# The second chunk's bonus on the diagonal of its scores, and its inverse scan fed from PSUM in two halves

## The chip, the core and the metric

The kernel runs on one core of a Trainium2 chip. The metric is the device time of one execution in microseconds (us), taken as the median of several executions. The core has a matrix engine (TensorE, PE in the rows; its weight loads are PEld), a vector engine (VectorE, DVE), a scalar engine (ScalarE, ACT), GpSimd (POOL), and SyncE (SP), whose queue issues the loads. They share an SBUF memory; TensorE writes to PSUM, which is in 8 banks and which VectorE and ScalarE can read and write too.

## The reference

Three layers in a row: a linear attention with decays and a bonus `u`, a dense ELU layer, and a layer of 4 experts.

```python
def _attn_ref(r, k, v, w, u):          # B, H, S, D = 2, 8, 768, 48
    for t in range(S):
        kt, vt, rt, wt = (k[:, :, t], v[:, :, t], r[:, :, t], w[:, :, t])
        cur = np.einsum('bhd,bhe->bhde', u[None] * kt, vt)
        y[:, :, t] = np.einsum('bhd,bhde->bhe', rt, state + cur)
        state = wt[:, :, :, None] * state + np.einsum('bhd,bhe->bhde', kt, vt)
...
def _moe_ref(x, w_in, w_out):          # 1536 tokens, 384 -> 2048 -> 384
    h = x @ w_in
    g = np.where(h > 0.0, h, alpha * (np.exp(np.minimum(h, 0.0)) - 1.0))
    return (g @ w_out).astype(np.float32)
...
def _moe2_ref(x, domain_probs, w1, w2):  # 4 experts, 384 -> 1024 -> 384
    p = domain_probs / (domain_probs.sum(-1, keepdims=True) + 1e-09)
    for e in range(E):
        h = np.maximum(x @ w1[e], 0.0)
        out += p[:, e:e + 1] * (h @ w2[e])
```

## The kernel before

The 1536 tokens are 12 chunks of 128. For a chunk, VectorE scans the decays forward (`products`, L840), takes the reciprocal of the last product of each of 8 segments (L843, `inv_end`), and scans backward from them (`inverses`, L849). The results scale k and r (`scale_k` L858, `scale_r` L865). TensorE makes the scores of 8 heads (`scores`, L1141) into two banks, one for even and one for odd heads; VectorE masks them into `att` (L878); TensorE multiplies `att` with v, first the even heads (L1220), then the odd ones (L1224, L1228), which gives the attention's output y, transposed. ScalarE rounds it into `x_hi` (L680, L689) and VectorE takes the remainder into `x_lo` (L907, L917). The matrix products of the layers are each three passes over such high and low parts (L1288 to L1290).

The bonus adds, to each token's y, its v times a number for each head: the sum over d of r, k and u. For chunks 2 to 11 that number is written on the diagonal of `att`: GpSimd multiplies r, k and u (L494, L498), VectorE sums them (L897), GpSimd writes the diagonal (`bonus_diagonal`, L506), and VectorE lays the masked scores beside it (L881). The first two chunks go another way: GpSimd multiplies r and k (L583), TensorE multiplies that with `u_blk`, in which `u` fills 48 columns for each head (`bonus`, L1182, 4 matmuls of 96 columns, each in two passes), VectorE multiplies v with the result (`bonus_v`, L903), and TensorE transposes this product into y (`turn_bonus`, L1195). `u_blk` is made by ScalarE (L704) from the 4 columns of `u_col`.

Chunks 0 and 1 stand ahead of everything; they are the tokens of the first, 256 wide tile of the ELU layer. This layer is a loop of steps n, 16 for each of 4 tiles. Step n makes 128 of the 2048 hidden values with `up(n)` (9 matmuls), ScalarE takes relu and exp (L737, L739), VectorE ends the ELU (`elu`, L953), ScalarE rounds (`hi_g`, L745), VectorE takes the remainder (`lo_g`, L959), and TensorE runs `down1(n)` two steps later, so its order is up(2), down1(0), up(3), down1(1) and so on. Between them come the later chunks, by tables of steps (`SCORES`, `PRODUCTS`, `SCALE_K` and so on): chunk 2's scores are in step 8, chunk 3's in step 12.

During the first tile the weights are rounded as well. Slice n (a tuple `(n, half)`: half 0 is for `up(n)`, half 1 for `down1(n)`) lands in `raw`; ScalarE makes `w_hi` (whole slices L693, halves L698 in the order of `HI_BETWEEN`), and the remainder `w_lo` is made by GpSimd (L517, two pieces of 192 columns for each half, in the order of `LO_POOL`) or by VectorE (L924, `LO_VECTOR`). `up(n)` waits for its slice's `w_lo`. GpSimd's order is fixed: the two r times k products, 11 halves (22 pieces), the bonus terms of chunk 2, the half (9, 0), the diagonal of chunk 2, five halves, the bonus terms of chunk 3, and so on. It begins the 22 pieces when chunk 1's r is scaled:

```python
            pool.wait_ge(s_qp, FIRST)
```

At the start TensorE also runs matmuls on zeros (`warm`, L1257; `fill`, L1262), which keep it busy and clear banks. After the four tiles come the experts, which TensorE runs through with the other engines feeding it.

## Time and profile before

| what | value |
|---|---|
| median of 3 executions | 652.43 us (652.41 to 652.44) |
| the profiled execution's own time | 652.4 us |
| its span in the trace | 650.6 us |
| granted TensorE clock, mean | 1.00 of full speed |
| TensorE matmul busy | 644.9 us (99%) |
| VectorE / ScalarE / GpSimd busy | 415.0 / 242.9 / 295.5 us |

The span is the time from the first to the last instruction in the trace; the execution's own time has 1.8 us around it. Busy time of TensorE counts matmuls from issue to modelled end, and they overlap, so a start time tells more than a share.

### The profile page before, as it was taken

To read this page: it belongs to the slowest core of one execution; us is meant where nothing else is said; L and a number is where in the kernel's file an instruction comes from. 1 tells how busy PE (TensorE), PEld (TensorE's weight loads), DVE (VectorE), ACT (ScalarE), POOL (GpSimd) and SP (SyncE) were. 2 spreads that over 40 slices of the span, in tenths; PEclk is the share of its full clock that TensorE was granted. 3 is DMA by queue.
4 is the path that set the end of the run, shared out by engine and by line. 5 is a ranking of instruction groups with operands and counts; after the bars stand their busy time and mean duration, and the time that the engine had idled before them with its cause. 6 is when DMAs were issued, how large, how long until landed. Compare 5 with 4: busy or idle time off the path is not lost.

```text
span 650.6 us, 13114 instructions
## 1 busy us (share of the span) xinstructions
PE 644.9 (99%) x4727; PEld 597.6 (92%) x4727; DVE 415.0 (64%) x775; ACT 242.9 (37%) x569; POOL 295.5 (45%) x370
## 2 busy tenths in 40 slices
PE   8999999999999999999999999999999999999998
PEld 5999999787888888999999999999999999999997
DVE  7888887865347666656565656565656565656564
ACT  4786656655435555322222222222222222222221
POOL 4897422520299999998009900009910019000000
PEclk9999999999999999999999999999999999999999
DMA  8933234200000133100012100013100011001011
GB/s 326 404 124 111 87 101 158 85 3 2 2 1 1 50 98 97 50 2 1 0 49 98 49 2 0 0 49 98 49 0 0 0 49 49 1 1 48 0 50 48
DMA packets 13280, 38.09 MB, mean 59 GB/s; under 512 B 1968, under 2 KB 4016, under 8 KB 13232
## 3 DMA queue, kind: packets, MB, share of 16 engines
q1 hardware_dynamic: 12944, 37.03, 16.2%
q8 instruction: 33, 0.54, 0.3%
q10 hardware_dynamic: 288, 0.39, 0.2%
q14 instruction: 15, 0.12, 0.1%
HBM read 35.06 MB, written 2.36 MB: 58 GB/s over the span
## 4 chain that ended last, share of the span: by engine, by line
PE 96%; DVE 2%; issue 1%; ACT 1%; DMA 0%; DVEq 0%; ACTq 0%
PE bank L1288 30%; PE bank L1289 30%; PE bank L1290 30%; PE bank L1141 2%; PE bank L1208 1%; PE bank L1220 1%; PE bank L1164 1%; PE bank L1152 1%; DVE fr L840 1%; DVE fr L849 0%; DMA rkw<-rkw_dram 0%; PE bank L1224 0%; PE bank L1228 0%; DVE bank L953 0%; PE bank L1195 0%
## 5 line engine op out<-in xcount | busy, mean ns | idle before, releaser
L1288 PE MATMUL bank<-x_lo,w_hi 128*128 128x256 f32 (+2 forms) x416 | 137.8, 331 | 0.0
L1289 PE MATMUL bank<-x_hi,w_lo 128*128 128x256 f32 (+2 forms) x416 | 135.2, 325 | 0.0
L1290 PE MATMUL bank<-x_hi,w_hi 128*128 128x256 f32 (+2 forms) x416 | 135.2, 325 | 0.0
L1289 PE MATMUL bank<-w_hi,g_lo 128*128 128x384 f32 x384 | 129.6, 337 | 0.0
L1290 PE MATMUL bank<-w_hi,g_hi 128*128 128x384 f32 x384 | 129.3, 337 | 0.0
L1288 PE MATMUL bank<-w_lo,g_hi 128*128 128x384 f32 x384 | 129.0, 336 | 0.0
L803 ACT ACTIVATE g_hi<-bank 128x512 fp32r<-128x512 f32 x96 | 57.5, 599 | 144.3 <-DVE bank L1009 122.4
L1288 PEld LDWEIGHTS bank<-x_lo,w_hi 128*128 128x128 f32 x416 | 78.3, 188 | 8.0 <-issue 0.4
L1290 PEld LDWEIGHTS bank<-x_hi,w_hi 128*128 128x128 f32 x416 | 78.2, 188 | 7.4
L1289 PEld LDWEIGHTS bank<-x_hi,w_lo 128*128 128x128 f32 x416 | 78.3, 188 | 7.1
L1002 DVE TENSOR_TENSOR u_sum<-p_copy,bank 128x256 f32<-128x256 f32 x56 | 23.6, 421 | 92.5 <-ACT p_copy L725 91.8
L529 POOL TENSOR_TENSOR raw<-raw 128x128 f32<-128x128 f32 x16 | 7.4, 463 | 157.7 <-DMA raw<-w_dram 157.7
L1288 PEld LDWEIGHTS bank<-w_lo,g_hi 128*128 128x128 f32 x384 | 72.2, 188 | 0.0
L1290 PEld LDWEIGHTS bank<-w_hi,g_hi 128*128 128x128 f32 x384 | 72.1, 188 | 0.0
L1289 PEld LDWEIGHTS bank<-w_hi,g_lo 128*128 128x128 f32 x384 | 72.0, 188 | 0.0
L725 ACT COPY p_copy<-bank 128x256 f32<-128x256 f32 x56 | 21.0, 375 | 134.4 <-PE bank L1290 134.3
L1082 DVE SCALAR_TENSOR_TENSOR g_lo<-bank,g_hi 128x512 fp32r<-128x512 f32 x96 | 65.9, 686 | 7.1 <-ACT g_hi L803 6.8
L1288 PE MATMUL bank<-g_lo,w_hi 128*128 128x256 f32 (+1 forms) x192 | 65.3, 340 | 0.2 <-DVE g_lo L959 0.2
L1290 PE MATMUL bank<-g_hi,w_hi 128*128 128x256 f32 (+1 forms) x192 | 64.9, 338 | 0.0
L1289 PE MATMUL bank<-g_hi,w_lo 128*128 128x256 f32 (+1 forms) x192 | 64.7, 337 | 0.0
L953 DVE SCALAR_TENSOR_TENSOR bank<-neg,bank 128x256 f32<-128x256 f32 (+1 forms) x64 | 35.9, 561 | 42.2 <-ACT neg L739 42.0
L541 POOL TENSOR_TENSOR w_lo<-raw,w_hi 128x768 fp32r<-128x768 f32 x32 | 58.6, 1853 | 0.0
(132 smaller groups left out, 1274.1 us busy)
## 6 DMA issues: line engine op xcount, KB each, us to landing
raw<-w_dram SPq DMA_DIRECT2D x48, 384.0 KB, 3.7
rkw<-rkw_dram SPq DMA_DIRECT2D x10, 772.5 KB, 5.2
tok<-tok_dram SPq DMA_DIRECT2D x10, 576.0 KB, 6.6
out_dram<-acc SPq DMA_DIRECT2D x10, 192.0 KB, 1.9
rkw<-rkw_dram SPq DMA_DIRECT2D x2, 512.0 KB, 4.1
rkw<-rkw_dram SPq DMA_DIRECT2D x2, 260.5 KB, 3.1
tok<-tok_dram SPq DMA_DIRECT2D x2, 192.0 KB, 4.9
out_dram<-acc ACTq DMA_DIRECT2D x2, 192.0 KB, 1.9
```

The costliest lines, as they stand in the source:

```text
L529: pool.tensor_tensor(s1, a21, a22, ALU.add).then_inc(s_ws, 1)
L541: pool.tensor_tensor(w_lo[:, slot, :], raw[:, slot, :], w_hi[:, slot, :].bitcast(F32), ALU.subtract).then_inc(s_w, 1)
L725: act.copy(p_copy[:, 0, :], bank[6][:, 0:QUARTER]).then_inc(s_pc, 1)
L803: act.activation(g2[0][:, p % 2 * 2 + o, :], bank[o][:, :], ACT.Relu).then_inc(s_gh, 1)
L840: dve.tensor_tensor_scan(fr[:, 0:SCAN], rkw[c % DEEP][:, 2 * NRK:2 * NRK + SCAN], reset[:, :], 0.0, ALU.mult, ALU.add).then_inc(s_f, 1)
L953: dve.scalar_tensor_tensor(out=h, in0=neg[:, k, 0:w], scalar=-1.0, in1=h, op0=ALU.add, op1=ALU.max).then_inc(s_elu, 1)
L1002: dve.tensor_tensor(u2, p1, p6, ALU.add).then_inc(s_u2, 1)
L1082: dve.scalar_tensor_tensor(out=g2[1][:, r, :], in0=bank[o][:, :], scalar=0.0, in1=g2[0][:, r, :].bitcast(F32), op0=ALU.max, op1=ALU.subtra ...
L1141: ins = pe.matmul(banks["x"][o][:, cols], k[rows, cols], q[rows, cols], start=True, stop=True)
L1288: pe.matmul(out, wh, ml, start=start, stop=False, skip_group_check=shared)
L1289: pe.matmul(out, wl, mh, start=False, stop=False, skip_group_check=shared)
L1290: return pe.matmul(out, wh, mh, start=False, stop=stop, skip_group_check=shared)
```

## The change

For chunk 1 the bonus goes on the diagonal of `att` too. TensorE's `bonus` now multiplies with `u_col` itself, which has 2 columns for each pair of heads (the 96 column blocks and `u_blk` are gone), so it yields 8 numbers for each token. ScalarE copies chunk 1's 8 numbers to `bonus_sb` and writes the four even heads' diagonals (`even_diagonals`); GpSimd writes the odd heads' ones in one instruction, ahead of its 22 pieces. VectorE then lays the masked scores beside them with four predicated copies of 256 columns in place of two multiplications of 512, the first two pairs of heads ahead of the last two; the scores of the last two pairs go to banks 6 and 7. `turn_bonus` and `bonus_v` remain for chunk 0 alone, and `values_by_block` follows the masks' order. Chunk 0's y keeps its way.

Chunk 1's reciprocals go to banks 0 and 1, and its inverse scan reads them there, in two scans of 260 columns. GpSimd's second r times k product now waits for the first of these only. Chunk 2's inverse scan, which was one scan at the end of step 3, becomes two, at the end of steps 3 and 4.

Slice 5's `w_hi` is no longer made whole ahead of the steps, but in halves in steps 0 and 1, and what followed moves by a half up to step 2. The order of GpSimd's first halves becomes (0, 0), (1, 0), (0, 1), (1, 1). The fills at the start are one more, and go to other banks.

```diff
-INVERSES = {FIRST: 3}
+FIRST_INVERSES = {FIRST: 3}
...
-LO_POOL = [(n, half) for n in range(J1) for half in range(2) if (n, half) not in LO_VECTOR + LO_LAST] + LO_LAST
+LO_AHEAD = [(0, 0), (1, 0)]
+LO_POOL = LO_AHEAD + [(n, half) for n in range(J1) for half in range(2)
+                      if (n, half) not in LO_AHEAD + LO_VECTOR + LO_LAST] + LO_LAST
...
-HI_FIRST = 6
-HI_BETWEEN = {1: ((6, 0), (6, 1)), 2: ((7, 0),), 3: ((7, 1), (8, 0)), 4: ((8, 1),), 5: ((10, 0),),
+HI_FIRST = 5
+HI_BETWEEN = {0: ((5, 0),), 1: ((5, 1), (6, 0)), 2: ((6, 1), (7, 0)), 3: ((7, 1), (8, 0)), 4: ((8, 1),), 5: ((10, 0),),
...
-            u_col = sb("u_col", [P, PAIRS], scope=scope)
-            u_blk = sb("u_blk", [P, PAIRS, PD], scope=scope)
+            u_col = sb("u_col", [P, PAIRS, 2], scope=scope)
...
-            bonus_v_sb = sb("bonus_v_sb", [P, 2, DM], scope=scope)
+            bonus_v_sb = sb("bonus_v_sb", [P, DM], scope=scope)
...
+        BANKS0 = dict(x=bank[6:8], y=bank[2], yt=blocks_in(bank[2]), kt=bank[5], u=heads_in(bank[6], 0),
+                      bonus=bank[3][:, P:P + H])
+        BANKS1 = dict(x=bank[0:2], x_late=bank[6:8], yt=[bank[b][:, 0:P] for b in (4, 3, 5)], kt=bank[7],
+                      u=heads_in(bank[7], 0), bonus=bank[5][:, P:P + H])
+
+        ENDS1 = bank[0:2]
...
         def inverted(c):
 
-            return c + 1 + max(c - FIRST, 0)
+            return 2 * c + 1
+
+        def ended(c):
+
+            return c + 1 + min(c, 1)
...
-            sp.dma_start(const[:, :], const_d).then_inc(s_const, 16)
+            sp.dma_start(const[:, :], const_d[:, 0:C_BLK]).then_inc(s_const, 16)
...
+            def on_diagonal(c, o):
+
+                heads = bonus_sb[:, c % 2, :].rearrange("p (a o) -> p o a", o=2)
+                return pool.affine_select(att[:, o, :, :], heads[:, o, :].unsqueeze(2).broadcast_to([P, PAIRS, CH]),
+                                          pattern=[[0, PAIRS], [1, CH]], compare_op=ALU.is_equal, fill=0.0, base=0,
+                                          channel_multiplier=-1)
...
+            pool.wait_ge(s_first_bon, 1)
+            pool.wait_ge(s_val, 1)
+            on_diagonal(1, 1).then_inc(s_diag_odd, 1)
             pool.wait_ge(s_qp, FIRST)
             def lo_ws(halves):
...
+
+            def even_diagonals(banks):
+                act.wait_ge(s_pb, 2)
+                act.copy(bonus_sb[:, 1, :], banks["bonus"]).then_inc(s_first_bon, 1)
+                act.wait_ge(s_val, 1)
+                act.wait_ge(s_const, 16)
+                act.wait_ge(s_first_bon, 1)
+                for p in range(PAIRS):
+                    act.activation(att[:, 0, p, :], ident, ACT.Copy,
+                                   scale=bonus_sb[:, 1, 2 * p:2 * p + 1]).then_inc(s_diag_even, 1)
+
             copy_tail(0)
-            act.wait_ge(s_uc, 32)
-            act.wait_ge(s_const, 16)
-            for p in range(PAIRS):
-                act.activation(u_blk[:, p, :], blocks, ACT.Copy, scale=u_col[:, p:p + 1]).then_inc(s_ub, 1)
             copy_kt(0, BANKS0)
...
             hi_w(1)
             copy_odd(1)
             hi_w(2)
+            even_diagonals(BANKS1)
             hi_w(3)
             hi_x(0, BANKS0["y"])
-            hi_w(4)
             for k in range(KT):
                 hi_x_block(1, BANKS1["yt"], k)
-            hi_w(5)
+            hi_w(4)
...
-                dve.reciprocal(inv_end[:, SEG - 1:SCAN:SEG], fr[:, SEG - 1:SCAN:SEG]).then_inc(s_end, 1)
+                if c == 1:
+                    dve.wait_ge(s_clear, 2)
+                    for ends, first in zip(ENDS1, (0, SCAN // 2)):
+                        dve.reciprocal(ends[:, SEG - 1:SCAN // 2:SEG],
+                                       fr[:, first + SEG - 1:first + SCAN // 2:SEG]).then_inc(s_end, 1)
+                else:
+                    dve.reciprocal(inv_end[:, SEG - 1:SCAN:SEG], fr[:, SEG - 1:SCAN:SEG]).then_inc(s_end, 1)
 
             def inverses(c, part=0, parts=1):
 
-                dve.wait_ge(s_end, c + 1)
+                dve.wait_ge(s_end, ended(c))
                 n = SCAN // parts
+                if c == 1:
+                    ends = backwards(ENDS1[1 - part], n - 1, TILE, n)
+                else:
+                    ends = backwards(inv_end, SCAN - 1 - part * n, SCAN, n)
                 dve.tensor_tensor_scan(backwards(fr, 2 * SCAN - 1 - part * n, 2 * SCAN, n),
                                        backwards(rkw[c % DEEP], 2 * NRK + SCAN - part * n, RKW, n),
-                                       backwards(inv_end, SCAN - 1 - part * n, SCAN, n), 0.0,
+                                       ends, 0.0,
                                        ALU.mult, ALU.add).then_inc(s_fr, 1)
...
+
+            def mask_half(o, late, banks):
+
+                if late:
+                    dve.wait_ge(s_px, 2)
+                else:
+                    dve.wait_ge(s_px_first, 1)
+                if o == 0:
+                    dve.wait_ge(s_diag_even, 2 * late + 2)
+                else:
+                    dve.wait_ge(s_diag_odd, 1)
+                pairs = slice(2 * late, 2 * late + 2)
+                masks = mask.unsqueeze(1).broadcast_to([P, 2, CH])
+                found = banks["x_late" if late else "x"][o][:, :].rearrange("p (a t) -> p a t", a=PAIRS)[:, pairs, :]
+                dve.copy_predicated(att[:, o, pairs, :], masks.bitcast(I32), found).then_inc(
+                    s_att if late else s_att_first, 1)
...
+            def bonus_v(banks):
+                dve.wait_ge(s_pb, 1)
+                landed(dve, s_tok, 0)
+                heads = v_of(0).rearrange("p (h d) -> p h d", h=H)
+                dve.tensor_tensor(bonus_v_sb[:, :].rearrange("p (h d) -> p h d", h=H), heads,
+                                  banks["bonus"].unsqueeze(2).broadcast_to([P, H, D]), ALU.mult).then_inc(s_cv, 1)
...
             products(1)
-            inverses(1)
+            inverses(1, 0, 2)
+            inverses(1, 1, 2)
             dve.wait_ge(s_const, 16)
             mask_scores(0, 0, BANKS0)
             mask_scores(0, 1, BANKS0)
             scale_k(1)
             scale_r(1)
-            bonus_v(0, BANKS0)
-            bonus_v(1, BANKS1)
-            mask_scores(1, 0, BANKS1)
-            mask_scores(1, 1, BANKS1)
+            bonus_v(BANKS0)
+            for late in range(2):
+                for o in range(2):
+                    mask_half(o, late, BANKS1)
...
-                for c in due(n, 0, INVERSES):
-                    inverses(c)
+                for part in range(2):
+                    for c in due(n, part, FIRST_INVERSES):
+                        inverses(c, part, 2)
...
                         rows, cols = slice(64 * o, 64 * o + D), slice(p * CH, (p + 1) * CH)
-                        ins = pe.matmul(banks["x"][o][:, cols], k[rows, cols], q[rows, cols],
-                                        start=True, stop=True)
+                        x = banks["x_late"] if c == 1 and p >= 2 else banks["x"]
+                        ins = pe.matmul(x[o][:, cols], k[rows, cols], q[rows, cols], start=True, stop=True)
+                    if c == 1 and p == 1:
+                        ins.then_inc(s_px_first, 1)
                 ins.then_inc(s_px, 1)
...
-                pe.wait_ge(s_ub, PAIRS)
-                if c == 1:
-                    pe.wait_ge(s_kt, 1)
+                pe.wait_ge(s_uc, 32)
                 for p in range(PAIRS):
-                    ins = pe.matmul(banks["bonus"][:, p * PD:(p + 1) * PD], rk[:, c, p * CH:(p + 1) * CH], u_blk[:, p, :],
-                                    start=True, stop=True)
+                    ins = pe.matmul(banks["bonus"][:, 2 * p:2 * p + 2], rk[:, c, p * CH:(p + 1) * CH], u_col[:, p, :],
+                                    start=False, stop=True, skip_group_check=True)
                 ins.then_inc(s_pb, 1)
...
+            def turn_bonus(yt):
+
+                pe.wait_ge(s_cv, 1)
                 for k in range(KT):
-                    ins = pe.matmul(yt[k], bonus_v_sb[:, c % 2, k * P:(k + 1) * P], ident,
-                                    start=first and (k == 0 or c == 1), stop=True, is_transpose=first,
+                    ins = pe.matmul(yt[k], bonus_v_sb[:, k * P:(k + 1) * P], ident, start=False, stop=True,
                                     skip_group_check=True)
-                if not first:
-                    ins.then_inc(s_py, 1)
+                ins.then_inc(s_py, 1)
...
+            def values_by_block(yt):
+
+                landed(pe, s_tok, 1)
+                pe.wait_ge(s_att_first, 1)
+                for b in (0, 1, 3, 4):
+                    even_strip(1, yt, b)
+                pe.wait_ge(s_att_first, 2)
+                pe.wait_ge(s_odd, 2)
+                odd_strip(1, yt, 2)
+                odd_end(1, yt, 1).then_inc(s_y_first, 1)
+                odd_strip(1, yt, 5)
+                odd_end(1, yt, 4)
+                pe.wait_ge(s_att, 3)
+                for b in (6, 9, 7, 10):
+                    even_strip(1, yt, b)
+                pe.wait_ge(s_att, 4)
+                odd_end(1, yt, 7).then_inc(s_y_first, 1)
+                odd_strip(1, yt, 8)
+                odd_strip(1, yt, 11)
+                odd_end(1, yt, 10).then_inc(s_py, 1)
...
             pe.wait_ge(s_zero, 2)
-            warm(WARM_UP, 1)
+            warm(WARM_UP // 2, 0)
+            warm(WARM_UP - WARM_UP // 2, 1)
             pe.wait_ge(s_zero, 4)
-            fill(2, 1)
+            fill(1, 3)
+            fill(1, 4)
             scores(0, BANKS0)
             pe.wait_ge(s_const, 16)
             turn_k(0, BANKS0)
             bonus(0, BANKS0)
-            fill(1, 1)
-            fill(1, 2)
+            fill(2, 2)
+            pe.wait_ge(s_kt, 1)
+            fill(1, 5)
             values_even(0, BANKS0["yt"])
             values_odd(0, BANKS0["yt"], s_val)
             bonus(1, BANKS1)
             scores(1, BANKS1)
-            turn_bonus(0, BANKS0["yt"], False)
-            turn_bonus(1, BANKS1["yt"])
-            values_even(1, BANKS1["yt"])
-            values_odd_by_block(1, BANKS1["yt"])
+            turn_bonus(BANKS0["yt"])
+            values_by_block(BANKS1["yt"])
             update(0, BANKS0)
```

ScalarE before the loop and in its step 0, before:

```order
L652 COPY tail<-fr 128x4
L704 ACTIVATE u_blk<-const,u_col 128x96 x4
L647 COPY kt_sb<-bank 128x512
L652 COPY tail<-fr 128x4
L676 COPY v_odd<-tok 128x4x16
L693 CAST w_hi<-raw 128x768 x2
L676 COPY v_odd<-tok 128x4x16
L693 CAST w_hi<-raw 128x768 x2
L680 CAST x_hi<-bank 128x3x128
L693 CAST w_hi<-raw 128x768
L689 CAST x_hi<-bank 128x128 x3
L693 CAST w_hi<-raw 128x768
```

And now, from the second copy of `v_odd` up to step 0's rounding of g:

```order
L696 COPY v_odd<-tok 128x4x16
L713 CAST w_hi<-raw 128x768
L723 COPY bonus_sb<-bank 128x8
L728 ACTIVATE att<-const,bonus_sb 128x128 x4
L713 CAST w_hi<-raw 128x768
L700 CAST x_hi<-bank 128x3x128
L709 CAST x_hi<-bank 128x128 x3
L713 CAST w_hi<-raw 128x768
L764 ACTIVATE neg<-bank 128x256
L766 ACTIVATE neg<-neg 128x256
L667 COPY kt_sb<-bank 128x512
L718 CAST w_hi<-raw 128x384
```

The four activations of 96 columns at the start are gone; a copy of 8 columns and four activations of 128 columns stand between slice 2 and slice 3; of slices 4 and 5, one whole cast is left behind the `x_hi` casts, and a half of slice 5 stands in step 0.

GpSimd from its first product to the diagonal of chunk 2, before:

```order
L583 TENSOR_TENSOR rk<-rkw 128x512 x2
L517 TENSOR_TENSOR w_lo<-raw,w_hi 128x192 x22
L494 TENSOR_TENSOR tok<-tok 128x192 x2
L498 TENSOR_TENSOR tok<-tok,u_rep 128x192 x2
L517 TENSOR_TENSOR w_lo<-raw,w_hi 128x192 x2
L506 AFFINE_SELECT att<-bonus_sb 128x512 x2
```

And now:

```order
L600 TENSOR_TENSOR rk<-rkw 128x512 x2
L517 AFFINE_SELECT att<-bonus_sb 128x512
L534 TENSOR_TENSOR w_lo<-raw,w_hi 128x192 x22
L507 TENSOR_TENSOR tok<-tok 128x192 x2
L511 TENSOR_TENSOR tok<-tok,u_rep 128x192 x2
L534 TENSOR_TENSOR w_lo<-raw,w_hi 128x192 x2
```

One diagonal of 512 columns stands ahead of the 22 pieces; all else keeps its place behind it.

## Rows read from the trace of the kernel before

**Rows 1.** The page's first part: busy time, share and instructions of each engine.

```profile
PE 644.9 (99%) x4727; PEld 597.6 (92%) x4727; DVE 415.0 (64%) x775; ACT 242.9 (37%) x569; POOL 295.5 (45%) x370
```

**Rows 2.** Windows, 60 to 640 us: busy time by engine, clock, DMA share, GB/s.

```profile
60.00:640.00 580.00, 580.00 (x4059) 539.32 (x4058) 360.19 (x674) 201.25 (x457) 248.11 (x302) 1.00 0.12 39
```

**Rows 3.** The chain that ended last, up to 18 us: start, us, what.

```profile
11.11 0.67 DVE att L878
...
11.92 0.65 PE bank L1220 x16
...
13.07 1.06 PE bank L1182 x8
14.13 1.09 PE bank L1141 x16
15.22 1.19 PE bank L1195 x9
...
17.43 0.60 PE bank L1164 x16
```

**Rows 4.** VectorE's timeline at the head: start, us, instruction, operands.

```profile
5.19 1.24 DVE L849 TENSOR_TENSOR_SCAN fr<-rkw,inv_end 128x520 f32<-128x520 f32 x1
...
9.31 1.88 DVE L849 TENSOR_TENSOR_SCAN fr<-rkw,inv_end 128x520 f32<-128x520 f32 x1
...
13.12 0.68 DVE L865 TENSOR_TENSOR neg<-rkw,fr 128x512 f32<-128x512 f32 x1
```

**Rows 5.** GpSimd's timeline at the head.

```profile
7.91 2.19 POOL L583 TENSOR_TENSOR rk<-rkw 128x512 f32<-128x512 f32 x1 [5.04 <-DVE neg L865]
...
13.88 18.33 POOL L517 TENSOR_TENSOR w_lo<-raw,w_hi 128x192 fp32r<-128x192 f32 x22 [1.23 <-DVE neg L865]
```

**Rows 6.** TensorE's timeline: the two fills behind the first bonus matmuls.

```profile
11.06 0.71 PE L1262 MATMUL bank<-g_hi 128*128 128x512 f32 x2
```

**Rows 7.** Groups up to 60 us, by form: count, busy us, mean ns, idle before.

```profile
L881 DVE COPY_PREDICATED att<-const,bank 128x512 f32<-128x512 int32 x4 | 2.7, 730 | 0.0
...
L667 ACT ACTIVATE st<-st,alpha 128x96 f32<-128x96 f32 x8 | 2.3, 368 | 0.0
...
L652 ACT COPY tail<-fr 128x4 f32<-128x4 f32 x4 | 0.8, 198 | 3.0 <-DVE fr L840 2.8
...
L506 POOL TENSOR_SCALAR_AFFINE_SELECT att<-bonus_sb 128x512 f32<-128x512 f32 x4 | 2.4, 633 | 0.7 <-DVE bonus_sb L897 0.7
```

**Rows 8.** ScalarE's timeline around the first `up`.

```profile
16.12 0.48 ACT L680 CAST x_hi<-bank 128x384 fp32r<-128x384 f32 x1 [1.50 <-PE bank L1195]
16.50 0.84 ACT L693 CAST w_hi<-raw 128x768 fp32r<-128x768 f32 x1
...
20.67 0.37 ACT L745 CAST g_hi<-bank 128x256 fp32r<-128x256 f32 x1
```

**Rows 9.** Groups up to 60 us, by form: the casts of half a slice.

```profile
L698 ACT CAST w_hi<-raw 128x384 fp32r<-128x384 f32 x20 | 9.4, 504 | 0.0
```

**Rows 10.** Timelines of VectorE, then TensorE, around chunk 2's inverse scan.

```profile
28.45 1.69 DVE L849 TENSOR_TENSOR_SCAN fr<-rkw,inv_end 128x520 f32<-128x520 f32 x1
...
31.04 0.42 DVE L959 TENSOR_TENSOR g_lo<-bank,g_hi 128x256 fp32r<-128x256 f32 x1
...
31.08 0.28 PE L1290 MATMUL bank<-x_hi,w_hi 128*128 128x256 f32 x1
31.52 0.39 PE L1288 MATMUL bank<-g_lo,w_hi 128*128 128x256 f32 x1 [0.16 <-DVE g_lo L959]
```

**Rows 11.** Groups up to 60 us, by form: the inverse scans of 260 columns.

```profile
L849 DVE TENSOR_TENSOR_SCAN fr<-rkw,inv_end 128x260 f32<-128x260 f32 x4 | 2.8, 692 | 0.0
```

**Rows 12.** Timelines of GpSimd, then TensorE: half (9, 0) and `up(9)`.

```profile
36.00 1.59 POOL L517 TENSOR_TENSOR w_lo<-raw,w_hi 128x192 fp32r<-128x192 f32 x2
...
38.53 0.36 PE L1288 MATMUL bank<-x_lo,w_hi 128*128 128x256 f32 x1
```

**Rows 13.** Timelines of VectorE, then TensorE: half (14, 0) and `up(14)`.

```profile
50.58 0.55 DVE L897 TENSOR_REDUCE bonus_sb<-tok 128x8 f32<-128x384 f32 x1 [1.04 <-POOL tok L498]
51.05 0.42 DVE L953 SCALAR_TENSOR_TENSOR bank<-neg,bank 128x256 f32<-128x256 f32 x1
...
52.24 0.59 DVE L924 TENSOR_TENSOR w_lo<-raw,w_hi 128x384 fp32r<-128x384 f32 x1
...
53.41 0.29 PE L1288 MATMUL bank<-x_lo,w_hi 128*128 128x256 f32 x1
```

61 lines of the change are left out of this document (20 added, 41 removed).

## The prediction, made before the changed kernel ran

> **What bounds the kernel now.** First the page's first part: TensorE is busy for 644.9 of the span's 650.6 us [rows 1], and a window from 60 to 640 us has it busy in all 580 us, at a granted clock of 1.00, the 2.4 GHz level [rows 2]. There the reader sees that nothing behind 60 us can be won or lost but by matmuls, and the change removes none there. So the change is worth exactly the time by which TensorE's stream of `up` and `down1` reaches its steady part earlier or later. Then the chain that ended last, for the head: it goes through VectorE's first mask at 11.11, and from 11.92 to the end of chunk 0's update at 18.03 it lies on TensorE [rows 3]. `up(0)` starts at 17.99. Third, the timelines of the four engines up to 60 us, to find every wait of TensorE in the loop. There are two short ones: 0.2 us before `down1(0)`, which waits for step 0's `lo_g`, and one at 31.08, where a matmul is followed by the next at 31.52 although they elsewhere follow in 0.12; it waited for the `lo_g` at 31.04, and this for the scan of 1.69 us at 28.45 [rows 10]. Last, the slices: by how much each `w_lo` is done before the `up` that waits for it. That is the view on which my number hangs.
>
> The profiled execution took 652.4 us, 1.8 more than its span; the median is 652.43. I count shifts of TensorE's stream and add them to 652.4.
>
> **The inverse scan of chunk 1.** A scan of 520 columns takes 1.24 us when GpSimd is idle (at 5.19) and 1.88 at 9.31 [rows 4], while GpSimd's first product runs from 7.91 to 10.10 [rows 5]. The excess is 0.64, and 9.31 + 0.64 is about where GpSimd ends. The Trainium skill (SBUF — State Buffer, section "SBUF: two separate sides") says that a VectorE instruction with two SBUF inputs and a GpSimd instruction that reads SBUF take turns on a port pair for a whole instruction each; by it, a scan fed from PSUM has one SBUF input and waits for nothing, and the trace's 0.64 agrees. No row shows a scan fed from PSUM. Bounds: with the excess gone, two halves of 0.69 as later ones [rows 11], less 0.08 of overlap, behind two reciprocals that cost 0.1 more than one: VectorE gets to the first mask at about 10.75 in place of 11.11. With the excess staying it is 11.3. I take the first, but it makes no difference worth a name, because of what TensorE does. It ran two fills from 11.06, the second at 11.38 [rows 6], and now runs three of about 0.21 (the distance at the full clock, from these rows between 0.2 and 0.3), so that it is not free before 11.8, and the switch to the narrow matmuls of `values_even` adds 0.1: 11.9, as before. The mask is ready by then in both cases. Only the odd half comes sooner, since it no longer waits for the second mask: 0.1. VectorE's earlier `scale_r` (it ended at 13.80 [rows 4], now about 13.2) releases chunk 1's scores, which however stand behind the bonus matmuls on TensorE.
>
> **The bonus matmuls.** Eight passes took 1.06 us with 96 columns [rows 3], 0.13 each; `turn_bonus` did nine passes of 128 columns in 1.19, 0.13 each as well. A quarter fewer columns saved nothing, so the weights, 128 columns in both, set the pace. With 2 columns I take no saving; the other bound is that nearly all of 1.0 us goes. The Trainium skill (TensorE: Matmul & The Clock Gate, section "LDWEIGHTS (loading the stationary operand)") gives the load of 128 columns as 107 ns whatever follows, which would leave at most 0.02 us a pass to win. So chunk 1's bonus ends at 14.03 (14.13 - 0.1) and its scores run from 13.95 to 15.1.
>
> **The diagonals and masks.** ScalarE copies the 8 numbers (0.2, as the small copy of 198 ns) to 14.2, then writes four diagonals. The nearest rows are activations of 96 columns, 368 ns each [rows 7], which follow each other in 0.27; 128 columns give 0.29 and 0.39. The second ends at 14.9, the fourth at 15.5. GpSimd's diagonal takes 0.63 [rows 7] from 14.3. VectorE's predicated copies of 512 columns take 0.73 [rows 7]; of 256 columns, 0.46, one each 0.36. They start at 14.9, 15.3, 15.5 and 15.9 and end at 16.35. Before, the masks ended at 16.56. TensorE drops three of nine passes of `turn_bonus`, 0.35 us, and reaches the last odd heads at 16.4, chunk 0's update at 16.8 and `up(0)` at 17.4 (the update took 0.60 [rows 3]). But `up(0)` also waits for x. ScalarE's cast of slice 3, 0.84 a piece [rows 8], now stands behind the diagonals, 15.4 to 16.2; the `x_hi` casts, which started at 16.12 [rows 8], start at about 16.15, and slice 4's cast between them is gone, so that the `x_lo` of the first block is there at 17.4 in place of 17.84. I take `up(0)` at 17.55: 0.44 earlier. Bounds: 0.1 (if the diagonals cost 0.1 more each) and 0.8.
>
> **Steps 0 to 4.** ScalarE now casts half of slice 5 in step 0, 0.50 us by the group [rows 9], 0.40 of it in the queue, between `copy_kt` and `hi_g(0)`, which stood at 20.67 [rows 8]. With 0.44 - 0.40 it stands at about 20.5 to 20.65, and `elu(1)` is 0 to 0.15 earlier. `lo_g(0)` waited for VectorE's `add_update` and is 0.4 earlier, which TensorE's `down1(0)` gets. From there TensorE has no wait up to 31.08, so its lead is 0.35. Then chunk 2's scan: one half of 0.69 [rows 11] leaves step 3, so `lo_g(4)` is there by 0.6 to 1.0 earlier than 31.04 and TensorE's stall of 0.32 (31.52 less 31.08 less 0.12), with 0.1 of slower restart, is gone [rows 10]. The second half stands behind `lo_g(4)`; `lo_g(5)` was done 0.7 us before `down1(5)`, which covers it; uncovered it would cost 0.6. TensorE's lead at step 8 is then 0.35 + 0.42, about 0.75 us.
>
> **GpSimd, and where the lead goes.** Its 22 pieces started at 13.88 [rows 5]. Now a diagonal stands ahead of them, which waits for TensorE's bonus and ScalarE's copy: start 14.3, 0.6 in the queue, pieces from 14.9. That is 1.0 late, and GpSimd has no idle time between 13.88 and 50.5 in which to catch up. The order in front gives (1, 0) earlier, so the first steps are safe: (3, 0) was 2.5 us ahead of its `up`, (7, 0) 2.1. But (9, 0) ends at 36.00 + 1.59 = 37.59 and `up(9)` starts at 38.53 [rows 12]: 0.94 of slack, against a lateness of 1.0 plus TensorE's lead of 0.75. TensorE will wait there, and what remains of the lead is 0.9 less the lateness. The second place is behind it: VectorE sits idle for 1.04 us until GpSimd has chunk 3's bonus terms, at 50.58, and from there `elu`, `hi_g`, `lo_g` and half (14, 0) follow one another, to 52.24 + 0.59 = 52.83; `up(14)` starts at 53.41 [rows 13]. Slack 0.58, less 0.05 to hand over: 0.53. A lateness L gives TensorE's stream a shift of L - 0.53, later, unless that is under minus 0.75. L starts at 1.0. It changes by chance: 22 pieces of 0.59 alone took 18.33, the rest being turns with VectorE's scans and remainders, and two half scans in place of a whole one save GpSimd perhaps 0.2. Bounds for L at 50 us: 0.3 and 1.2. I take 0.65, so the shift is +0.1 and the time 652.5.
>
> **Rivals.**
> - The lead is carried (chance 0.27). GpSimd's lateness shrinks to 0.3 or less, because the bonus matmuls with 2 columns do come cheaper and its diagonal starts at 13.9, or because its turns with VectorE fall well. For it: what these turns cost it is a matter of phase (18.33 us against 22 x 0.67 [rows 5]). Time 652.4 - 0.2 to 0.8, 651.6 to 652.2.
> - Slower through GpSimd (0.16). L is 1.0 or more at 50 us. The mechanism is the one place `up(14)`, the price is L - 0.53, and it decides from L = 0.53 on; beyond 0.2% it needs L above 1.8, for which the diagonal would have to start at 15.1. Time 652.9 to 653.3.
> - The change does not do what it says (0.07): diagonals dearer than 0.5 us each put the masks at 17, `up(0)` is not earlier, only the stall at 31 goes, and GpSimd is late in addition. Time 652.3 to 653.
> - The forecast (0.50): `up(9)` and `up(14)` take the lead back; 652.2 to 652.8.
>
> **How the numbers follow.** A measurement of this kernel tells 0.2% from no change, 1.3 us, so the bounds are 651.1 and 653.7. The largest gain that the head and the stall hold is 0.8 + 0.42 = 1.2 us, still inside; the loss needs L above 1.8. So: same 0.93, faster 0.03, slower 0.04. The range for 8 in 10 takes the forecast and most of both neighbours: 651.6 to 653.0. Its lower end is the whole lead carried, 652.4 - 0.75, its upper end L of 1.1.
>
> **What the profile would show.** `values_even` of chunk 0 at 11.9 still, behind a third fill; eight bonus passes still near 1.0 us; an inverse scan of 260 columns at 9.4 with no excess; masks ending near 16.35; `up(0)` near 17.55; `hi_g(0)` near 20.6; no gap at 31. GpSimd's 22 pieces from 14.9; a wait of TensorE before `up(9)`, for GpSimd, and one before `up(14)`, for VectorE. If TensorE waits at neither, I am wrong in L and the time is below 652. If `up(0)` is at 18 or later, I am wrong in the diagonals.

## The result, and the profile after

The changed kernel takes 653.41 us, the median of 20 executions (653.12 to 655.03), against 652.45 us for the kernel before, measured beside it (20 executions, 652.35 to 652.54). The ratio is 1.0017, with a 95% interval of 1.001 to 1.0023. That is 0.96 us more, still inside the 0.2% named in the prediction, but outside its range, and the forecast was 652.5.

The first profiled execution took 654.88 us and had a low TensorE clock for 3.4 us at the head (it is shown further down, for its clock). The rows of this section are from another execution of the same kernel, with the clock at 1.00: 653.35 us, span 651.5, where before had 652.4 and 650.6.

First the page's first part and the window from 60 to 640 us. They answer to [rows 1] and [rows 2].

```profile
PE 645.1 (99%) x4725; PEld 597.8 (92%) x4725; DVE 414.7 (64%) x779; ACT 243.3 (37%) x571; POOL 295.9 (45%) x371
...
60.00:640.00 580.00, 579.95 (x4058) 539.03 (x4058) 360.54 (x675) 201.48 (x457) 248.99 (x303) 1.00 0.12 39
```

TensorE reads as full behind 60 us, as before, but for 0.05 us. Waits of 0.1 or 0.2 us hide under the modelled ends in this view, so the starts are read from here on. TensorE's timeline at the head:

```profile
10.20 1.05 PE L1238 MATMUL bank<-u_col,rk 128*128 128x2 f32 x8 [0.59 <-POOL rk L600]
11.12 0.96 PE L1328 MATMUL bank<-g_hi 128*128 128x512 f32 x3
12.00 0.64 PE L1268 MATMUL bank<-att,tok 128*32 128x128 f32 x16
...
14.00 1.16 PE L1198 MATMUL bank<-neg,tok 48*128 48x128 f32 x16
...
17.24 0.67 PE L1222 MATMUL bank<-tok,kt_sb 128*64 128x48 f32 x16
17.84 0.39 PE L1355 MATMUL bank<-x_lo,w_hi 128*128 128x256 f32 x1
```

From the start of chunk 1's eight bonus passes to the start of its scores it is 0.98 us now (13.02 to 14.00), where it was 1.06 with 96 columns [rows 3]: 0.08 less for eight passes. (The 1.05 in the row counts the last pass to its modelled end.) Chunk 0's values start at 12.00 behind three fills. Chunk 0's update starts 0.12 earlier than before, at 17.24 for 17.36 on the same timeline, and `up(0)` starts at 17.84, only 0.15 before the 17.99 of before. VectorE, then ScalarE, then GpSimd at the head:

```profile
9.41 1.28 DVE L886 TENSOR_TENSOR_SCAN fr<-rkw,bank 128x260 f32<-128x260 f32 x2
10.61 1.26 DVE L912 TENSOR_TENSOR att<-bank,const 128x512 f32<-128x512 f32 x2
...
15.18 1.45 DVE L931 COPY_PREDICATED att<-const,bank 128x256 f32<-128x256 int32 x4 [1.65 <-ACT att L728]
```
```profile
14.11 0.17 ACT L723 COPY bonus_sb<-bank 128x8 f32<-128x8 f32 x1 [0.73 <-PE bank L1238]
14.39 1.28 ACT L728 ACTIVATE att<-const,bonus_sb 128x128 f32<-128x128 f32 x4
```
```profile
7.96 3.60 POOL L600 TENSOR_TENSOR rk<-rkw 128x512 f32<-128x512 f32 x2 [5.08 <-DVE neg L902]
...
14.34 0.63 POOL L517 TENSOR_SCALAR_AFFINE_SELECT att<-bonus_sb 128x512 f32<-128x512 f32 x1 [2.79 <-ACT bonus_sb L723]
14.95 5.17 POOL L534 TENSOR_TENSOR w_lo<-raw,w_hi 128x192 fp32r<-128x192 f32 x7
```

The two scans fed from PSUM take 1.28 us together, from 9.41, while GpSimd's products run from 7.96 to 11.56; in their place stood 1.88 [rows 4]. The masks end at 15.18 + 1.45 = 16.63. GpSimd's 22 pieces start at 14.95, 1.07 us later than at 13.88 [rows 5]. GpSimd, VectorE and TensorE where the prediction saw its two waits:

```profile
37.20 1.25 POOL L534 TENSOR_TENSOR w_lo<-raw,w_hi 128x192 fp32r<-128x192 f32 x2
```
```profile
51.45 0.55 DVE L948 TENSOR_REDUCE bonus_sb<-tok 128x8 f32<-128x384 f32 x1 [1.59 <-POOL tok L511]
51.92 0.42 DVE L1008 SCALAR_TENSOR_TENSOR bank<-neg,bank 128x256 f32<-128x256 f32 x1
52.78 0.42 DVE L1014 TENSOR_TENSOR g_lo<-bank,g_hi 128x256 fp32r<-128x256 f32 x1 [0.44 <-ACT g_hi L772]
53.12 0.59 DVE L978 TENSOR_TENSOR w_lo<-raw,w_hi 128x384 fp32r<-128x384 f32 x1
```
```profile
38.60 0.36 PE L1355 MATMUL bank<-x_lo,w_hi 128*128 128x256 f32 x1 [0.25 <-POOL w_lo L534]
...
53.86 0.36 PE L1355 MATMUL bank<-x_lo,w_hi 128*128 128x256 f32 x1 [0.23 <-DVE w_lo L978]
```

Half (9, 0) ends at 38.46 (37.20 + 1.25 in the rounded row), 0.87 later than at 37.59 [rows 12]; `up(9)` waits for it, and starts 0.07 later than before. VectorE waits for chunk 3's bonus terms until 51.45, 0.87 later than before [rows 13], and `up(14)` waits for the remainder behind it: 53.86 in place of 53.41, 0.45 later. But the kernel ends 0.9 later. The other 0.44 us are lost behind `up(14)`. TensorE there, before the change and then after it:

```profile
62.16 0.28 PE L1290 MATMUL bank<-g_hi,w_hi 128*128 128x256 f32 x1
62.37 0.49 PE L1141 MATMUL bank<-rkw 48*128 48x128 f32 x4
...
67.86 0.32 PE L1288 MATMUL bank<-g_lo,w_hi 128*128 128x256 f32 x1
68.01 0.28 PE L1289 MATMUL bank<-g_hi,w_lo 128*128 128x256 f32 x1
```
```profile
62.76 0.28 PE L1357 MATMUL bank<-g_hi,w_hi 128*128 128x256 f32 x1
63.09 0.38 PE L1198 MATMUL bank<-rkw 48*128 48x128 f32 x2
...
68.47 0.28 PE L1357 MATMUL bank<-g_hi,w_hi 128*128 128x256 f32 x1
68.67 0.39 PE L1355 MATMUL bank<-g_lo,w_hi 128*128 128x256 f32 x1
```

And what they wait for on VectorE (`scale_r` of chunk 4, a remainder of x), before and after:

```profile
61.47 0.68 DVE L865 TENSOR_TENSOR rkw<-rkw,fr 128x512 f32<-128x512 f32 x1
...
67.32 0.41 DVE L969 TENSOR_TENSOR x_lo<-bank,x_hi 128x256 fp32r<-128x256 f32 x1
```
```profile
62.35 0.69 DVE L902 TENSOR_TENSOR rkw<-rkw,fr 128x512 f32<-128x512 f32 x1
...
68.22 0.39 DVE L1024 TENSOR_TENSOR x_lo<-bank,x_hi 128x256 fp32r<-128x256 f32 x1
```

Three places behind `up(14)` add to it. The first is the second tile's first `up`, which waits for the x of chunk 3: VectorE ended it at 59.72 before, 0.43 ahead of the `up` at 60.15, and ends it at 60.60 now; the `up` starts at 60.65, and the matmul behind it 0.61 later than before. Chunk 4's scores started 0.21 us behind the matmul ahead of them before the change, which is what such a change of tile takes elsewhere too (36.39 to 36.60 in the changed kernel), and start 0.33 behind it now. Their `scale_r` ended at 62.15 before, 0.2 ahead of them, and ends at 63.04 now; so this place lets 0.72 of the lateness through (63.09 for 62.37). At 68 us a remainder of x on VectorE ended at 67.73, ahead of the matmul at 67.86, and now ends at 68.61, ahead of one at 68.67. That start is 0.81 later, the restart costs 0.1 more (68.89 for 68.01), and from there on every start is 0.88 to 0.89 later.

### The profile page after: what moved, and what is told of

Read it like the earlier page. It is cut to its first block, busy times and chain, and to the rows that moved or that the text cites. A ratio compares the mean times of both kernels' runs of the same rounds, so it can differ in the third digit from the quotient of the medians.

```text
span 653.0 us, 13118 instructions
## 1 busy us (share of the span) xinstructions
PE 646.5 (99%) x4725; PEld 598.7 (92%) x4725; DVE 414.6 (63%) x779; ACT 243.3 (37%) x571; POOL 295.7 (45%) x371
## 4 chain that ended last, share of the span: by engine, by line
PE 91%; POOL 4%; DVE 2%; issue 1%; ACT 1%; DMA 0%; POOLq 0%; DVEq 0%; ACTq 0%
PE bank L1355 29%; PE bank L1356 28%; PE bank L1357 28%; POOL w_lo L534 3%; PE bank L1198 2%; PE bank L1262 1%; PE bank L1268 1%; PE bank L1222 1%; PE bank L1210 1%; DVE fr L867 0%; DMA rkw<-rkw_dram 0%; PE bank L1284 0%; PE bank L1280 0%; PE bank L1238 0%; POOL rk L600 0%
```

## The experiments

Each of the twelve runs was timed against the kernel before in the same measurement (medians of 11 or 12 executions; the kernel before 652.45 to 652.51). The times given are medians; the ratios are of means, so a few long executions move them. A ratio's interval reaches some 0.6 us to either side or more, so only experiments 1, 3, 8 and 9 are clear of no change by it. Smaller differences rest on the rows, and on the other executions of a kernel mostly lying within 0.1 to 0.3 us of its median.

**1. The same kernel again.** Nothing is edited.

> The changed kernel, unaltered, for a second profile. Theory (GpSimd's lateness): the median is again near 653.4, and in an execution whose granted clock is 1.00 all through, GpSimd's 22 pieces start about 1.0 us later than before (near 14.9), TensorE waits for GpSimd's half (9, 0) at up(9) and for VectorE's half (14, 0) at up(14), each with under 0.2 us between the half's end and the up. Rival (the head): up(0) itself is 0.9 us later than before even without a fall of the clock, and the later slack is as before. Rival (the clock): every execution has a stretch at 1.2 GHz near 11 to 15 us and it makes the loss.

653.41 us (653.28 to 654.88), ratio 1.0017 (1.0008 to 1.0026). The rows above are from it: the pieces at 14.95, both waits of TensorE, and `up(0)` not later than before, with the clock at 1.00. That is the first theory, and it leaves the other two out. The 0.96 us are no property of one measurement.

**2. GpSimd's diagonal away.** VectorE multiplies the identity with the 4 odd numbers in one instruction ahead of its predicated copies.

```diff
-            on_diagonal(1, 1).then_inc(s_diag_odd, 1)
...
+                dve.tensor_tensor(att[:, 1, :, :], ident.unsqueeze(1).broadcast_to([P, PAIRS, CH]),
+                                  heads.unsqueeze(2).broadcast_to([P, PAIRS, CH]), ALU.mult).then_inc(s_diag_odd, 1)
```

> The changed kernel with the odd heads' diagonals made by VectorE (one multiplication of 512 columns, about 0.7 us, at 14.2, when VectorE is idle) in place of GpSimd. GpSimd's 22 pieces then start with the end of chunk 1's scale_r, near 13.1. Theory (lateness): no wait at up(9) and up(14) is left, TensorE's lead is carried, and the time is 651.6 to 652.2 in executions without a fall of the clock. Rival (the head): at most 0.1 us faster than the changed kernel.

652.17 us (651.98 to 653.86), ratio 1.0003 (0.9994 to 1.0012). GpSimd's pieces start at 13.1, half (9, 0) ends 0.76 earlier than before the change, and `up(14)` is at 53.12. To take one instruction of 0.63 us, and the wait ahead of it, out of GpSimd's queue is worth 1.24 us.

**3. Only a late GpSimd.** The kernel before, with two clearings of an unused tile ahead of the 22 pieces, and nothing of the change.

```diff
+            for i in range(2):
+                need(pool, s_pad, i)
+                pool.memset(pad[:, :], 0.0).then_inc(s_pad, 1)
```

> The kernel before, with two clears of an unused tile (512 columns each) on GpSimd ahead of its 22 pieces, about 1.1 us, and nothing else. Theory (lateness): up(9) and up(14) wait, and the time is later by 1.1 less 0.53 to 1.1 less 0.3, that is 0.6 to 0.8 us: 653.0 to 653.2. Rival (the head): 652.4 to 652.6.

653.59 us (653.29 to 653.75), ratio 1.0018 (1.0008 to 1.0027).

```profile
13.84 1.11 POOL L589 MEMSET pad<- 128x512 f32 x2 [1.21 <-DVE neg L870]
14.91 5.16 POOL L519 TENSOR_TENSOR w_lo<-raw,w_hi 128x192 fp32r<-128x192 f32 x7
...
37.34 1.25 POOL L519 TENSOR_TENSOR w_lo<-raw,w_hi 128x192 fp32r<-128x192 f32 x2
```

The pieces start at 14.91, half (9, 0) ends 1.0 later than before, and the span is 651.6, 1.0 longer. By the prediction's rule (lateness less 0.53) it would have been 0.5 longer, and the median is above the 653.0 to 653.2 expected. So a late GpSimd alone is enough for the whole loss, and is passed on in full.

**4. Only the split scan of chunk 2.** The kernel before with its inverse scan in two halves, at the ends of steps 3 and 4.

```diff
-INVERSES = {FIRST: 3}
+FIRST_INVERSES = {FIRST: 3}
...
-                for c in due(n, 0, INVERSES):
-                    inverses(c)
+                for part in range(2):
+                    for c in due(n, part, FIRST_INVERSES):
+                        inverses(c, part, 2)
```

> The kernel before, with chunk 2's inverse scan in two halves, at the end of steps 3 and 4, and nothing else. Theory: the gap at 31 us goes and 0.3 to 0.45 us are won at up(8); half (9, 0) had 0.94 us of slack and (14, 0) 0.58, so it is carried: 652.0 to 652.15. Rival: the second half delays a later step and nothing is won.

652.16 us (652.08 to 652.22), ratio 0.9996 (0.9987 to 1.0005). `up(8)` starts 0.39 earlier, as the prediction had it (0.42), and GpSimd's half (9, 0) 0.29 earlier; the end is 0.3 earlier. TensorE's lead is cut to that of GpSimd.

**5. The diagonal behind one half.** The changed kernel with half (0, 0) ahead of GpSimd's diagonal.

```diff
+            pool.wait_ge(s_qp, FIRST)
+            lo_w(*LO_POOL[0])
             pool.wait_ge(s_first_bon, 1)
             pool.wait_ge(s_val, 1)
             on_diagonal(1, 1).then_inc(s_diag_odd, 1)
-            pool.wait_ge(s_qp, FIRST)
...
-            lo_ws(LO_POOL[:before[0]])
+            lo_ws(LO_POOL[1:before[0]])
```

> The changed kernel with GpSimd's diagonal of chunk 1 placed behind its first half (0, 0) instead of ahead of it, so that GpSimd starts its pieces when chunk 1's r is scaled (near 13.1 us) and not at 14.95. Theory: the loss comes from GpSimd's lateness L against before, carried to the end with slope 1 (L 0.87 at half (9, 0) gave +0.89 at the end). The diagonal then fills no idle time, and what was idle from 13.1 to 14.95 does two pieces of work; its odd diagonal comes at 14.3 to 14.9. I expect half (9, 0) to end between 37.2 and 37.8 (before 37.59) and the end at 652.0 to 652.5. Rival: the loss is in the front part of the loop or in the masks themselves (a later up(0), the half cast of slice 5 in step 0), not in GpSimd's queue: then 653.2 to 653.6, as the change.

652.34 us (652.16 to 652.43), ratio 0.9998 (0.9989 to 1.0007).

```profile
13.21 1.26 POOL L534 TENSOR_TENSOR w_lo<-raw,w_hi 128x192 fp32r<-128x192 f32 x2 [1.60 <-DVE neg L903]
14.42 0.64 POOL L517 TENSOR_SCALAR_AFFINE_SELECT att<-bonus_sb 128x512 f32<-128x512 f32 x1
```

The same instructions in another order win back 1.07 us. Two pieces now stand where GpSimd was idle for the diagonal, which itself starts only 0.08 later than in the change. The rival, a loss in the masks or in step 0, is out: `up(0)` is at 17.89 and `up(8)` at 34.41, against 17.84 and 34.38 in the changed kernel.

**6. Slice 5 whole again.** Experiment 2 with slice 5's `w_hi` made whole ahead of the loop.

```diff
-HI_FIRST = 5
-HI_BETWEEN = {0: ((5, 0),), 1: ((5, 1), (6, 0)), 2: ((6, 1), (7, 0)), 3: ((7, 1), (8, 0)), 4: ((8, 1),), 5: ((10, 0),),
+HI_FIRST = 6
+HI_BETWEEN = {1: ((6, 0), (6, 1)), 2: ((7, 0),), 3: ((7, 1), (8, 0)), 4: ((8, 1),), 5: ((10, 0),),
```

> The changed kernel with the odd diagonals by VectorE (as the run that did this alone, 652.17 us) and slice 5 cast whole ahead of the loop again, as before the change. Theory: with GpSimd out of the way the end goes by TensorE's own lead, and the half cast of slice 5 in step 0 holds it back: lo_g(1) came 0.16 to 0.25 us later than before relative to nothing gained. I expect lo_g(1) 0.3 to 0.5 us earlier than with the half cast, up(8) 0.1 to 0.3 earlier, and 651.85 to 652.1. Rival: the whole casts delay x_hi ahead of the loop by as much, up(0) is 0.3 to 0.4 later, and the time stays 652.1 to 652.3.

651.95 us (651.88 to 652.15), ratio 0.9992 (0.9984 to 1.0001). `lo_g(1)` is 0.39 earlier and `up(8)` 0.28 earlier than in experiment 2. `up(0)` is at 17.82, where it was at 17.76. So half a cast in step 0 cost about what the prediction gave it (0.40).

**7. Two more warm-up matmuls.** Experiment 2 with `WARM_UP = 7`.

> The changed kernel with the odd diagonals by VectorE and two more warm-up matmuls at the start. Of 11 runs of that kernel without them three took 653.8 us in place of 652.1, and of 31 runs of the changed kernel four took 654 to 655; the one in the trace has the granted clock at the 1.2 GHz level from 11.5 to 14.9 us, before up(0). Theory C2 (TensorE's idle time at 7 to 8 us and its late start): no run above 653 in some 10, and the median 652.0 to 652.2. Theory C1 (the bonus matmuls with 2 columns keep TensorE's array too little at work, between 10.5 and 14 us): one to four runs in 10 still at 653.5 to 654.

652.43 us (652.08 to 653.0), ratio 1.0 (0.9992 to 1.0009). No execution is above 653.0, but six of 11 are spread from 652.4 to 653.0, where experiment 2 had eight within 651.98 to 652.19 and three at 653.8. Theory C2 has its first sign (none above 653) and not its second (the median), C1 has none; why the times are spread is open, and the run decides between neither.

**8. Only the narrow bonus matmuls.** The kernel before with `u_col` of 2 columns in place of `u_blk`, and the product with v reading 8 numbers.

```diff
-                    ins = pe.matmul(banks["bonus"][:, p * PD:(p + 1) * PD], rk[:, c, p * CH:(p + 1) * CH], u_blk[:, p, :],
+                    ins = pe.matmul(banks["bonus"][:, 2 * p:2 * p + 2], rk[:, c, p * CH:(p + 1) * CH], u_col[:, p, :],
```

> The kernel before with one part of the change: the bonus of chunks 0 and 1 multiplied with the 2 columns of u for each pair of heads instead of the 96 column blocks, and VectorE's product with v reading 8 numbers for each token. Nothing else. Theory: a pass costs the same with 2 columns as with 96 (0.13 us), so the median is that of before, 652.3 to 652.5. Theory C1 (the narrow matmuls bring the falls of the clock): one or more of some 11 runs at 653.8 to 654.5, where none of 53 runs of before was. Theory C2: none of them. Rival on the cost: passes are cheaper than the weights of 128 columns, values and scores come 0.3 us or more sooner and the time is below 652.2.

652.92 us (652.64 to 657.24), ratio 1.0025 (1.001 to 1.0041). Four of 12 executions took 655.8 to 657.2, with a mean clock of 0.992 to 0.995. The eight passes start 0.98 us ahead of the scores (13.09 to 14.07) where it was 1.06, so they are 0.08 cheaper, about as foreseen; the median, 0.45 above before, was foreseen by neither theory. Half (9, 0) ends 0.66 late; experiment 10 has the rows where that begins. One more thing overturns a reading: chunk 2's scan, here still whole, took 1.24 us (at 28.43) in place of 1.69, and `up(8)` is 0.38 earlier without any split. So the stall at 31 that the split takes away came of a turn with GpSimd too.

**9. The sum of chunk 3 moved.** The changed kernel with VectorE's sum of chunk 3's bonus terms behind step 12's `lo_g`.

```diff
+SUM_LATER = 12
...
+                if n == SUM_LATER:
+                    bonus(3)
                 for half in LO_AFTER.get(n, ()):
                     lo_w(*half)
                 for c in due(n, -1):
-                    bonus(c)
+                    if c != 3:
+                        bonus(c)
```

> The changed kernel with one instruction of VectorE moved: the sum of chunk 3's bonus terms (L948), for which VectorE stood idle for 1.59 us at 50 us with step 12's elu and lo_g behind it, now stands behind them in step 12. Theory: GpSimd's lateness of 0.87 us reaches TensorE only through what is queued behind this sum (elu, lo_g, half (14, 0), chunk 4's scan, chunk 3's masks). Then half (14, 0) is done 0.8 us or more sooner, TensorE's wait of 0.39 us before up(14) goes, as do the small ones behind it, and the end is that of up(9), 0.05 to 0.2 later than before: 652.45 to 652.7. Rival: GpSimd's lateness comes through other places as well (its late diagonal of chunk 3, chunk 3's masks, half (15, 0)): then up(14) is early, but a wait at 56 to 69 us takes its place and the time stays 653.1 to 653.4.

652.95 us (652.71 to 657.52), ratio 1.0013 (1.0001 to 1.0024). VectorE, then TensorE:

```profile
51.77 0.54 DVE L949 TENSOR_REDUCE bonus_sb<-tok 128x8 f32<-128x384 f32 x1
...
60.85 1.07 DVE L896 TENSOR_TENSOR rkw<-rkw,fr 128x512 f32<-128x512 f32 x1
61.85 1.08 DVE L903 TENSOR_TENSOR rkw<-rkw,fr 128x512 f32<-128x512 f32 x1
```
```profile
62.37 0.28 PE L1361 MATMUL bank<-g_hi,w_hi 128*128 128x256 f32 x1
62.99 0.38 PE L1202 MATMUL bank<-rkw 48*128 48x128 f32 x2 [0.34 <-DVE rkw L903]
```

The wait before `up(14)` is gone (53.62). In its place stands one of 0.4 us before chunk 4's scores, at 62.99: VectorE reached `scale_k` and `scale_r` 0.9 earlier, and there met GpSimd's bonus terms of the same chunk, so that they took 1.07 and 1.08 each, where the changed kernel has 0.69 for either. The span is 651.2. It is neither theory: the path through the sum is real, and about half the gain from clearing it is lost again to turns with GpSimd.

**10. The same with 64 columns.** Experiment 8, with 62 columns of zeros beside the 2 of u. The product with v picks its 8 numbers out of the wider blocks; all else stays.

```diff
+UW = 64
...
-            u_col = sb("u_col", [P, PAIRS, 2], scope=scope)
+            u_col = sb("u_col", [P, PAIRS, UW], scope=scope)
```

> The kernel before with only its bonus matmuls changed, as the run that gave 652.92 us and four of 12 executions at 655.8 to 657.2, but with 64 columns for each pair of heads (2 with numbers of u, 62 of zeros) in place of 2. Everything else is as there. Theory C1 (the matmuls of 2 columns bring the falls of the clock): no execution above 653.5 in some 11. Rival (ScalarE's missing activations or the broadcast product bring them, or chance): two or more of 11 at 655 to 657. For GpSimd either value of L is possible, since it hangs on how its turns with VectorE fall; median 652.4 to 653.0, and equal to before plus the lateness of half (9, 0) where that is above 0.

652.57 us (652.52 to 652.67), ratio 1.0002 (0.9993 to 1.001), and no execution is above 652.7. Beside experiment 8 it also shows how half a microsecond hangs on a tenth. GpSimd and VectorE at 18.2 us, first with 2 columns, then with 64:

```profile
18.20 1.87 POOL L517 TENSOR_TENSOR w_lo<-raw,w_hi 128x192 fp32r<-128x192 f32 x2
...
18.19 1.43 DVE L922 TENSOR_TENSOR w_lo<-raw,w_hi 128x384 fp32r<-128x384 f32 x2
```
```profile
18.14 1.48 POOL L518 TENSOR_TENSOR w_lo<-raw,w_hi 128x192 fp32r<-128x192 f32 x2
...
18.19 1.84 DVE L923 TENSOR_TENSOR w_lo<-raw,w_hi 128x384 fp32r<-128x384 f32 x2
```

GpSimd's pieces began at 13.98 in the one and at 13.91 in the other. At 18.2 VectorE is first in the one (18.19 before 18.20) and GpSimd in the other (18.14 before 18.19), and the one that comes second takes 0.4 longer: GpSimd's two pieces 1.87 in place of 1.48, VectorE's two halves 1.84 in place of 1.43. Further turns fall otherwise after it, and half (9, 0) ends at 38.25 and 37.65. The Trainium skill (SBUF — State Buffer, section "Who interferes with whom") says that a VectorE instruction with two SBUF inputs contends with a GpSimd instruction that reads SBUF, that their shared ports are an exclusive lock, and that the issue order decides who blocks; these rows agree.

**11. One fill fewer.** Experiment 6 with two fills, not three, ahead of chunk 0's values.

```diff
-            fill(2, 2)
+            fill(1, 2)
```

> The kernel with VectorE's odd diagonals and slice 5 cast whole ahead (651.95 us) with one fill fewer, two in place of three, ahead of chunk 0's values. It tests the step of the prediction that the third fill hides what the scan fed from PSUM gains. If it does, values_even of chunk 0 starts at 11.7 in place of 12.0, chunk 1's bonus and scores are 0.2 to 0.3 earlier, and so are the masks and up(0) (17.55 to 17.65 in place of 17.82). At the end it can show at most what GpSimd allows, whose half (9, 0) was 0.53 ahead of before: 651.75 to 651.95. Rival: chunk 1's scores wait for something else (VectorE's scale_r, ScalarE's queue), up(0) stays within 0.1 of 17.82, and TensorE idles instead.

651.98 us (651.86 to 656.4), ratio 1.0004 (0.999 to 1.0019); two of 12 executions at 656.4, with a mean clock of 0.991.

```profile
11.75 0.65 PE L1274 MATMUL bank<-att,tok 128*32 128x128 f32 x16
...
13.75 1.16 PE L1204 MATMUL bank<-neg,tok 48*128 48x128 f32 x16
...
17.59 0.38 PE L1361 MATMUL bank<-x_lo,w_hi 128*128 128x256 f32 x1
```

Values, scores and `up(0)` are each 0.22 or 0.23 earlier than in experiment 6. So the third fill did hide what the PSUM-fed scan had gained. At the end nothing of it is left: TensorE's lead at `up(8)` is 0.74, GpSimd's 0.54, and the span is 650.1 in both.

**12. All that the runs pointed to.** Experiment 11 with the sum moved as in 9 and bonus matmuls of 64 columns.

> All that the runs point to, together: the changed kernel with the odd diagonals by VectorE, slice 5 cast whole ahead, two fills, the sum of chunk 3's bonus terms behind step 12's lo_g, and bonus matmuls of 64 columns. Theory: the end goes by TensorE's own lead at up(8) (0.55 with three fills, up to 0.8 with two), since GpSimd's place is taken off the path: 651.6 to 651.9, with no execution above 653. Rival: the sum's move brings nothing on top where GpSimd is ahead anyhow, and the time is that of the kernel with three fills, 651.9 to 652.1.

652.08 us (652.01 to 652.69), ratio 0.9995 (0.9986 to 1.0003): not better than experiment 6, and above the 651.6 to 651.9 expected. TensorE's lead was 0.77 as late as the second tile's first `up`, at 59.38; then the two scalings of chunk 4 again took 1.07 and 1.09 (59.86 and 60.85), its scores started at 61.99 for 62.37, and 0.4 remained.

## Why the prediction was wrong

All kernels side by side, from their profiles. Each number is the start or end in that kernel less the one in the kernel before (34.80, 37.59, 50.54 and a span of 650.6); less is earlier. The spans are rounded to 0.1 us before they are subtracted.

| kernel | `up(8)` starts | half (9, 0) ends | chunk 3's bonus terms end | span |
|---|---|---|---|---|
| the change | -0.42 | +0.87 | +0.88 | +0.9 |
| 3 late GpSimd | -0.07 | +1.01 | +1.02 | +1.0 |
| 8 narrow | -0.38 | +0.66 | +0.66 | +0.6 |
| 10 64 columns | +0.04 | +0.06 | +0.14 | +0.1 |
| 5 half first | -0.38 | -0.20 | -0.18 | -0.2 |
| 4 split scan | -0.39 | -0.29 | -0.26 | -0.3 |
| 2 VectorE's diagonal | -0.27 | -0.76 | -0.36 | -0.3 |
| 7 warm-up | -0.24 | -0.69 | -0.32 | -0.3 |
| 6 slice 5 whole | -0.55 | -0.53 | -0.49 | -0.5 |
| 11 one fill fewer | -0.74 | -0.54 | -0.52 | -0.5 |
| 9 sum moved | -0.27 | +1.01 | +1.03 | +0.6 |
| 12 all | -0.76 | -0.72 | -0.70 | -0.4 |

But for the two in which the sum was moved, the span follows the fourth column within 0.1 us, and that column is the later of the two to its left, again within 0.1. So the end goes by when chunk 3's bonus terms are there, and these by TensorE's lead or by GpSimd's queue, whichever is later. What TensorE gained ahead of `up(8)` plays no part where GpSimd is late.

- **What was right.** The fills that hide the PSUM-fed scan, shown by experiment 11; bonus passes whose cost the columns hardly change (from the passes' start to the scores' start 0.98 us with 2 columns, 1.04 with 64, 1.06 with 96); the half cast's 0.4 (experiment 6); that the split takes the stall at 31 away (experiment 4; the stall itself hung on a turn, experiment 8); the start of the pieces, 14.9; the waits of TensorE at `up(9)` for GpSimd and at `up(14)` for VectorE.
- **The step that failed** is "A lateness L gives TensorE's stream a shift of L - 0.53". The slack at `up(14)` was read nearly right: with L at 0.87 its start moved by 0.45, where the rule gives 0.34, since the wait hands over 0.15 behind the half's end (53.71 to 53.86) and not 0.05. But it was taken for the slack of the whole queue behind the late sum. VectorE's queue goes on. Its later waits, of 0.44 and 0.28 us up to 60 us, are for ScalarE, which waited for VectorE's own `elu`, so that they made nothing up: up to 69 us every instruction of VectorE behind the sum starts 0.86 to 0.91 later than before. And the later readers of that queue had less slack: 0.4 us at the second tile's first `up`, 0.2 at chunk 4's scores and 0.1 at 68 us, and the slower restarts took the rest. In these kernels the rule is L, not L - 0.53: experiment 3 gave +1.0 at L of 1.0, and experiment 8 +0.6 at 0.66. This is 0.53 us of the error.
- **The size of L.** 0.65 was taken from a range of 0.3 to 1.2; it was 0.87. I had counted 0.2 for the halved scans, and about 0.15 for luck; the turns gave back 0.2 in all. Experiments 8 and 10 suggest that such a term can't be had to better than half a microsecond from a profile: they began 0.07 us apart and ended 0.6 apart. This is 0.22 of the error. The forecast's own shift was 0.1, and 0.1 + 0.53 + 0.22 is 0.85 of the 0.9 measured.
- **The diagonals** were late: ScalarE's copy ran at 14.11 and its first diagonal at 14.39, where 14.2 was taken, and VectorE's four copies started at 15.18 in place of 14.9. They took the 1.45 us foreseen, the masks ended at 16.63 for 16.35, and `up(0)` gained 0.15 for 0.44. So the lead at `up(8)` was 0.42 where 0.75 was foreseen: the head and step 0 together gave next to nothing (`up(6)` is 0.09 earlier than before), and all of the lead is the stall at 31. It cost nothing at the end, since GpSimd takes the lead anyhow.
- **The rivals.** "Slower through GpSimd", with a chance of 0.16, named the engine and the place, and had the price of L - 0.53 in it as well, so that it gave 652.9 at an L of 1.0. What came was its mechanism at an L of 0.87 and with a dearer price.

Left open: why GpSimd's lateness of 1.07 at its first piece becomes 1.72 at the 22nd and 0.87 at half (9, 0). The rows show turns with VectorE all the way, but which of them differ by the change and which by chance was not separated.

## What to carry to other kernels

When an instruction on which an engine waits comes later, don't read the slack at the next reader only. Follow that engine's queue for as long as it waits for nothing but what it set off itself, and take the smallest slack of all who wait for anything in it. And before an instruction is put at the head of a long queue, ask what the queue would do while it waits: one half ahead of the diagonal was worth 1.07 us here, where the best of all these kernels is 0.5 ahead of the kernel before.
